# The rank sums of group i-2 move between the second and the third convolution of group i

## The reference

```python
# 1: causal convolution over 7 taps, one softmaxed set of taps for each of 8 heads of 24 columns
w = softmax(weight)                                   # 8 x 7
out[b, s, head] = sum_k w[head, k] * x_pad[b, s + k, head]
# 2: mixture with skip: a token with x @ w_skip > 0 goes to the expert of the largest gate logit
y = gate * (relu(x @ w1[e]) @ w2[e]);  x = x + y      # the others are passed on unchanged
# 3: second mixture: logits get a bias by the token's modality; every token has one expert
out = gate * (relu(x @ w1[e]) @ w2[e])
```

## Time and profile before

| | |
|---|---|
| median of three runs | 1245.24 us (1243.87 to 1250.37) |
| the profiled execution | 1245.14 us, span 1243.5 us |
| mean granted clock of TensorE | 0.915 of full |
| busy | TensorE 1156.7 us (93%), VectorE 625.6 (50%), ScalarE 489.1 (39%), GpSimd 466.0 (37%) |

### The profile page before, as it was taken

One profiled execution on the slowest core, in us unless ns is written; L12 is line 12 of the kernel. 1 busy time (PEld: TensorE's weight loads), 2 busy tenths in 40 slices (PEclk: granted clock), 3 DMA queues, 4 the chain that ended last, 5 costly groups with the idle time before them and its releaser, 6 DMA issues. The chain is left out here.

```text
span 1243.5 us, 27561 instructions
## 1 busy us (share of the span) xinstructions
PE 1156.7 (93%) x8677; PEld 1136.5 (91%) x8678; DVE 625.6 (50%) x1896; ACT 489.1 (39%) x879; POOL 466.0 (37%) x576
## 2 busy tenths in 40 slices
PE   6999997499999999999965999999999999999997
PEld 5989997399999999999955999999999999999997
DVE  2665566145756566656673444444444444444444
ACT  4654553234444344443423333333333333333333
POOL 5576667233333332332323323322333232223324
PEclk8776665579999999999987999999999999999999
DMA  5444433544242414414123311111111111111110
GB/s 150 116 135 123 115 104 117 156 119 125 61 120 73 125 44 137 126 53 140 44 90 85 108 42 39 39 45 40 39 42 42 39 39 39 46 39 39 42 42 27
DMA packets 85580, 97.91 MB, mean 79 GB/s; under 512 B 26738, under 2 KB 76230, under 8 KB 85554
## 3 DMA queue, kind: packets, MB, share of 16 engines
q1 hardware_dynamic: 68362, 67.04, 20.3%
q0 software_dynamic: 15072, 28.47, 6.8%
q10 hardware_dynamic: 2120, 2.09, 0.5%
HBM read 65.79 MB, written 33.54 MB: 80 GB/s over the span
## 5 line engine op out<-in xcount | busy, mean ns | idle before, releaser
L893 PE MATMUL p_h<-xt,w_up 128*128 128x256 f32 x3600 | 461.9, 286 | 15.6 <-ACT xt L965 9.4
L893 PEld LDWEIGHTS p_h<-xt,w_up 128*128 128x128 f32 x3600 | 449.2, 191 | 20.6 <-ACT xt L965 11.7
L906 PE MATMUL p_y<-w_dn,hid_hi 128*128 128x384 f32 (+1 forms) x1440 | 446.7, 371 | 0.4 <-DVE hid_lo L1084 0.4
L986 ACT ACTIVATE hid_hi<-p_h 128x512 fp32r<-128x512 f32 x360 | 214.6, 597 | 515.5 <-PE p_h L893 514.1
L902 PE MATMUL p_y<-w_dn,hid_lo 128*128 128x192 f32 (+1 forms) x1440 | 352.2, 255 | 0.0
L1084 DVE SCALAR_TENSOR_TENSOR hid_lo<-p_h,hid_hi 128x512 fp32r<-128x512 f32 x360 | 247.2, 690 | 208.5 <-ACT hid_hi L986 208.0
L902 PEld LDWEIGHTS p_y<-w_dn,hid_lo 128*128 128x128 f32 x1440 | 276.1, 192 | 0.0
L906 PEld LDWEIGHTS p_y<-w_dn,hid_hi 128*128 128x128 f32 x1440 | 272.3, 189 | 1.4 <-DVE hid_lo L1084 0.6
L840 POOL DMA_INDIRECT out<-y_out,idx x114 | 112.3, 985 | 244.0 <-DVE y_out L1077 223.5
L833 POOL TENSOR_TENSOR split<-ahead,split 128x256 fp32r<-128x256 f32 x94 | 64.6, 687 | 303.1 <-ACT split L969 303.1
L432 POOL DMA_INDIRECT buckets<-rows,idx x128 | 126.2, 986 | 68.9 <-issue 48.5
(11 more groups left out here) (193 smaller groups left out, 1305.0 us busy)
## 6 DMA issues: line engine op xcount, KB each, us to landing
ahead<-buckets SPq DMA_DIRECT2D x94, 202.0 KB, 2.4
x_in<-in_x SPq DMA_DIRECT2D x16, 672.0 KB
stage<-in_w SPq DMA_DIRECT2D x11, 768.0 KB
kept<-buckets SPq DMA_DIRECT2D x33, 202.0 KB, 2.5
stage<-in_w SPq DMA_DIRECT2D x11, 512.0 KB
stage<-in_w SPq DMA_DIRECT2D x22, 256.0 KB
x_in<-in_w_t SPq DMA_DIRECT2D x9, 512.0 KB, 7.4
x_in<-in_w_t SPq DMA_DIRECT2D x9, 256.0 KB, 8.8
```

The source lines that it names most:

```text
L893: mm = nc.tensor.matmul(o, w_up[:, slot, w, f * P:(f + 1) * P], xt[:, a * UNIT:(a + 1) * UNIT], start=(m == 0), stop=(m == len(terms) - 1))
L906: mm = nc.tensor.matmul(p_y[:, t, 0:2 * COLS], hid_hi[:, f, c], w_dn[:, slot, f, :, 0:COLS], start=(f == 0), stop=(f == FT - 1))
L986: nc.scalar.activation(hid_hi[:, 2 * b:2 * b + 2, :], p_h[:, b % HB, :].rearrange("p (f c) -> p f c", f=2), ACT.Relu).then_inc(hi_done, 1)
```

## The change

In TensorE's `step` the call of `ranks(i - 2, ...)` moves from behind the fourth convolution to between the second and the third. No other engine's list and no other line is changed.

```diff
                         conv(i, b, k, 1)
+                        if not static or i >= 2:
+                            ranks(i - 2, b, (k - 2) % GB)
                         conv(i, b, k, 2)
                         if not static or i >= 1:
                             transpose(i - 1, b, (k - 1) % GB, 1)
                         conv(i, b, k, 3)
-                        if not static or i >= 2:
-                            ranks(i - 2, b, (k - 2) % GB)
                         if not static or i >= 1:
                             logits(i - 1, b, (k - 1) % GB)
```

## The result

| | before | after |
|---|---|---|
| median, first comparison (4 runs each) | 1244.55 us | 1252.85 us |
| ratio, 95% interval | | 1.0057 [1.0029, 1.0085] |
| median, second comparison (35 and 12 runs) | 1246.34 us | 1256.02 us |
| ratio, 95% interval | | 1.0073 [1.0041, 1.0105] |
| profiled execution, its span | 1245.14, 1243.5 us | 1253.98, 1252.2 us |

The change makes the kernel slower, by 8.3 us in the first comparison of medians and 9.7 in the second; both intervals exclude no change. Forecast were 1253 us and +7.8.

A forecast was written before the change was run, and what follows sets the result against it. TensorE's pace in steps 2 to 15 was taken to set the convolution stage's end. Lateness of 5.8 us plus net clock terms of 2.0 gave +7.8 on 1245.1, forecast 1253 us, range 1236 to 1262.

The forecast's parts named there:

- What bounds the stage: Convolution stage: TensorE's pace in steps 2 to 15 decides; it ends 30.7 us after group 13's row numbers are known.
- What gets earlier: VectorE's waits for ranks, 11.3 us in 8: step 12's row numbers 1.4 us earlier, but gains lost in later waits.
- The wait that is added: TensorE ahead of the third convolution, for `pick`: about 2 us in steps 3, 6, 10; about 1 in 2, 14.
- Step 2's expected wait: TensorE's wait for `pick` in step 2, at half clock: 1.0 us.
- The sum at an unchanged clock, +5.8: TensorE's lateness from added waits and later `pick`, less gaps in steps 4, 7, 11 that hide some: +5.8 us.
- The clock's fall, +4.3 each in two of three steps: TensorE falls to half clock after 2 us waits in two of steps 3, 6, 10: +8.6 us.
- The clock's return in steps 7 and 11, -3.3 each: With the gap for ScalarE filled, TensorE's clock rises in steps 7 and 11: -6.6 us.
- Rivals 1: Clock holds through the 2 us waits and rises in steps 7 and 11: -0.8, 1244 us; chance 0.22.
- 2 (the clock rises in steps 4, 8, 12): Ranks keep TensorE dense, clock rises there, -3.8 us each: -12.2 in all, 1233 us; chance 0.15.
- Rival 4: Three clock falls in steps 3, 6, 10 and no rise in 7, 11: +18.7, 1264 us; chance 0.05.
- Rival 3: TensorE's clock never falls and GpSimd runs without a wait: -18.5, 1227 us; chance 0.08.
- My bound of 1 us: The mixtures' part of the span, behind the convolution stage, was to move by no more than 1 us.

The follow-up runs named there:

- the wait alone: Kernel before with only TensorE's wait for `pick_done` added between the second and third convolution, ranks left behind the fourth; 1249.72 us, ratio 1.0034.
- filled step 6: Changed kernel with 18 matmuls on constants ahead of the ranks in steps 6, 10 and 14, filling TensorE's wait; 1256.59 us, ratio 1.0085.
- the second profile: The changed kernel profiled once more, with no further edit; ratio 1.0073 to the kernel before, last scatter at 232.82.
- the last candidate: Kernel before with ranks ahead of the fourth convolution and ScalarE's exponentials ahead of the third convolution's read; 1280.49 us against 1281.99, ratio 0.9997.

## Why the prediction was right

*What bounds the stage.* Right: the mixtures' part moved by 0.8 us in the pair of profiles, and the stage's end by 9.5. Of these, 2.75 us stood ahead of step 2, for which the forecast had no term; the first scatter came 3.4 us later instead of the forecast 1.4. The last wait of GpSimd was again in step 15, 29.4 us ahead of the last scatter.

*What gets earlier.* Right: VectorE's 11.3 us for the ranks were gone and nothing was gained. The kernel with the ranks before the fourth convolution shows it more cleanly: 10 us of that wait removed, ratio 0.9996.

*The wait that is added.* Right in place and size where TensorE arrived at full clock: 2.14 and 2.15 us against 2.03. In sum 9.5 us in six waits against 8.1 in five. Step 2's expected wait did not come; steps 7 and 11, for which I had none, had 0.89 each, probably because `pick` was later too behind a later step 6 or 10. The experiment with the wait alone shows that such a wait costs time (+4.6 us).

*The sum at an unchanged clock, +5.8.* No experiment isolates it. The wait alone gave +4.6, with what the clock did in it; filled step 6 puts the wait itself at 2.2 us a step (10.0 against 7.8).

*The clock's fall, +4.3 each in two of three steps.* Right in direction; the size is not the kernel's but the execution's. From the ranks to the last logit, the stretch priced in the prediction at 5.1 us, steps 3, 6 and 10 took 6.5 us each in the first profile: the clock fell in all three (in step 3 ahead of the wait already) and was back before the step's end, three times 1.4 us, 4.2 against 8.6. In the second profile the same stretch took 9.3, 8.2 and 6.5 us, 8.7 in sum above full clock.

*The clock's return in steps 7 and 11, -3.3 each.* Transposes, fourth convolution and logits took 7.5 us in both steps before. In the first profile they took 4.8 and 7.5, -2.7 in sum against -6.6: step 7 rose, step 11 did not. (The whole of step 7 shrank by 3.6 us, since its gap of 2.04 went too and a wait of 0.89 came.) In the second profile they took 4.7 and 4.1, -6.2 in sum.

The two clock terms together are thus +1.5 and +2.5 us in the two profiles, against +2.0. In the first, two errors of about 4 us with opposite signs cancelled, and that is luck; in the second both terms came out as priced. The kernel before isn't the same in every execution either: in its second profile steps 10 and 11 took 13.9 and 9.7 us instead of 8.3 and 14.2. So the forecast of the sum can be held to the runs, and that of single steps can't.

*The rivals.* Rivals 1 (the terms cancel) and 2 (the clock rises in steps 4, 8, 12) did not come: in the first profile these steps took 15.5, 15.5 and 15.9 us. Rival 4's three falls came, but not at its price of 4.3 us each, and with a return in step 7 or in both. Rival 3 (the clock never falls) did not come either: waits of 2.14 and 2.24 us were followed by a fall within some 1.5 us, and the same stretch with the wait filled was not. It would have followed from a rule of the Trainium skill ("TensorE: Matmul & The Clock Gate", section "HAM oscillation — how this bites in real kernels"), by which only a standstill longer than these sends the clock back; for this kernel the measurement decides against it.

What stays open: whether the ranks' matmuls ahead of the exponentials cost a part of their own (1.0018 and 1.0014, both within reach of 1), how much of the loss is the waits, and what sends the clock down behind the logits while TensorE is busy.

## What to carry to other kernels

A wait that is removed from an engine off the path can be worth nothing (here 10 us of VectorE's, ratio 0.9996), and a wait placed in the list of the engine that sets the pace costs up to its full length, where no gap behind it takes it up: before moving work earlier in an in-order list, compare the moment at which its input is written with the moment at which the list arrives, in the fastest step and not in the mean one. Here a place 2 us further on had the input ready. And where TensorE's clock moves between its levels, a wait can cost more than it lasts, here 3.6 and 5.4 us in step 6 for 2.14 us of waiting.

## What the runs showed that was not expected

The part behind the last scatter, in which no kernel differs, took from 1011.9 to 1026.2 us in thirteen profiles (the last candidate's left out), more than the whole effect of the change. The fastest and the slowest, from the last scatter to the end:

```profile
222.02:1233.90 1011.88, 953.92 (x7390) 942.27 (x7390) 502.39 (x1438) 381.94 (x704) 325.15 (x415) 0.98 0.24 69
```

```profile
229.30:1255.50 1026.20, 965.92 (x7390) 954.93 (x7390) 503.19 (x1438) 381.89 (x704) 324.78 (x415) 0.96 0.24 68
```

The number of matmuls is equal; the granted clock is 0.98 against 0.96, and TensorE's busy time differs by 12.0 of the 14.3 us. My bound of 1 us for this part was far too narrow: it held for the first pair of profiles by chance. For the same reason a difference between single runs says little about a change in the stage.
